# Weaving the first block's products between the last tiles of y, and the second batch's sums into later blocks

## The reference

```
mask   = q_bucket == k_bucket            # 6-bit hash of q and of k
attn   = softmax(where(mask, q @ k.T / 8, -1e9))
x      = attn @ v, put together to 1536 x 512
y      = max(x @ w1, x @ w2, x @ w3) @ moe_w_out      # 1536 x 512
h      = y @ w_in                        # 512 x 2048
g      = h * sigmoid(1.702 * h)
out    = g @ w_out2                      # 1536 x 512
```

## Time and profile before

| | us |
|---|---|
| median of three runs | 686.61 |
| the profiled execution, its own time | 686.38 |
| its span in the trace | 684.6 |
| TensorE busy | 667.9 |
| GpSimd busy | 467.9 |
| VectorE busy | 484.1 |
| ScalarE busy | 345.0 |

### The profile page before, as it was taken

How to read it: one execution, slowest core, us unless ns; L and a number is a source line. 1 busy time by engine, 2 the same in 40 slices (tenths; PEclk the granted TensorE clock), 3 DMA queues, 4 the chain that set the end, 5 groups by cost and what they waited for, 6 DMA issues and landing times.

```text
span 684.6 us, 11930 instructions
## 1 busy us (share of the span) xinstructions
PE 667.9 (98%) x3874; PEld 577.6 (84%) x3874; DVE 484.1 (71%) x971; ACT 345.0 (50%) x755; POOL 467.9 (68%) x539
## 2 busy tenths in 40 slices
PE   7899999999999999999999999899999999999998
PEld 5677776767777789999999999788888898898986
DVE  5877788787878799869788862866655556545454
ACT  3777877777777731011104344554455555544433
POOL 4756756688985899968861438977776667777510
PEclk9999999999999999999999999999999999999999
DMA  4835737548243101111100200322222214222102
GB/s 114 199 85 139 169 91 171 130 116 185 64 117 118 33 31 32 32 32 33 46 25 24 93 1 31 83 71 63 68 86 63 63 46 170 62 73 77 36 1 92
DMA packets 58700, 54.12 MB, mean 79 GB/s; under 512 B 28944, under 2 KB 47632, under 8 KB 58640
## 3 DMA queue, kind: packets, MB, share of 16 engines
q1 hardware_dynamic: 58320, 53.36, 29.0%
q10 hardware_dynamic: 320, 0.01, 0.0%
HBM read 32.51 MB, written 3.15 MB: 52 GB/s over the span
## 4 chain that ended last, share of the span: by engine, by line
PE 83%; POOL 6%; DVE 5%; ACT 2%; issue 2%; DMA 1%; SPq 0%; ACTq 0%; DVEq 0%; POOLq 0%
PE psS L1299 9%; PE psO L1321 9%; PE psR L1307 9%; PE psR L1368 6%; PE psR L1367 6%; PE psR L1369 6%; PE psS L1367 6%; PE psS L1368 6%; PE psS L1369 6%; PE psS L1488 3%; PE psS L1487 3%; PE psS L1486 3%; POOL w_lo L676 2%; PE psR L1268 2%; POOL w_parts L681 2%
## 5 line engine op out<-in xcount | busy, mean ns | idle before, releaser
L547 POOL TENSOR_SCALAR probs<-probs,lone,inv 128x768 f32<-128x768 f32 x96 | 93.7, 982 | 60.7 <-DVE inv L997 60.7
L676 POOL TENSOR_TENSOR w_lo<-w_raw,w_hi 128x256 fp32r<-128x256 f32 x96 | 78.3, 823 | 39.3 <-ACT w_hi L875 38.6
L979 DVE TENSOR_REDUCE neg_max<-psS 128x1 f32<-128x768 f32 x96 | 91.2, 951 | 12.3 <-PE psS L1299 9.1
L732 ACT ACTIVATE probs<-psS,neg_max 128x768 f32<-128x768 f32 x96 | 86.5, 901 | 20.9 <-DVE neg_max L979 20.9
L522 POOL TENSOR_SCALAR w_hi<-w_raw 128x256 fp32r<-128x256 f32 (+1 forms) x79 | 48.6, 618 | 48.4 <-PE psS L1369 26.9
L1307 PE MATMUL psR<-ident,probs 128*128 128x128 f32 x576 | 74.7, 273 | 2.5 <-ACT w_raw L725 0.9
L741 ACT ACTIVATE probs_t<-psR 128x384 f32<-128x384 f32 x128 | 59.5, 491 | 31.3 <-PE psR L1307 31.3
L1307 PEld LDWEIGHTS psR<-ident,probs 128*128 128x128 f32 x576 | 66.6, 140 | 7.1 <-POOL probs L547 3.7
L1321 PE MATMUL psO<-probs_t,v_raw 128*64 128x384 f32 x384 | 68.8, 494 | 0.0
L1202 DVE TENSOR_TENSOR v_raw<-psR,early 128x384 f32<-128x384 f32 x64 | 35.6, 556 | 39.9 <-PE psR L1369 39.2
L1367 PE MATMUL psR<-x_hi,w_hi 128*128 128x384 f32 x160 | 54.2, 339 | 4.6 <-POOL w_lo L676 3.8
(11 more groups left out here) (258 smaller groups left out, 1876.0 us busy)
## 6 DMA issues: line engine op xcount, KB each, us to landing
w_raw<-in_moe_w_in SPq DMA_DIRECT2D x16, 512.0 KB, 3.5
w_raw<-in_moe_w_out SPq DMA_DIRECT2D x32, 256.0 KB, 2.7
w_raw<-in_moe_w SPq DMA_DIRECT2D x9, 512.0 KB, 3.8
h_lo<-w_hi SPq DMA_DIRECT2D x22, 192.0 KB, 3.6
h_hi<-w_hi SPq DMA_DIRECT2D x18, 192.0 KB, 3.4
w_raw<-in_q SPq DMA_DIRECT2D x16, 192.0 KB, 3.4
w_raw<-in_k SPq DMA_DIRECT2D x16, 192.0 KB, 4.1
v_raw<-in_v SPq DMA_DIRECT2D x16, 192.0 KB, 2.5
```

What stands on the lines that cost most here:

```text
L547: pool.tensor_scalar(probs[i % PROBS][:, :], probs[i % PROBS][:, :], lone[:, i % 6:i % 6 + 1], inv[:, i % 6:i % 6 + 1], ALU.add, ALU.mult) ...
L676: pool.tensor_tensor(in2_slot(w_lo, n, which), in2_raw(n, PARTS2[which]), f32(in2_slot(w_hi, n, which)), ALU.subtract).then_inc(in2_split, 1)
L732: act.activation(probs[i % PROBS][:, :].rearrange("p (a b) -> p a b", a=2), psS[i % 2][:, :, 0:HALF], ACT.Exp, bias=neg_max[:, i % 6:i % 6 ...
L979: dve.tensor_reduce(neg_max[:, i % 6:i % 6 + 1], psS[i % 2][:, :, 0:HALF], AX.XY, ALU.min).then_inc(max_ready, 1)
```

## The change

Four things are moved; no computation is added or taken away, the work on each engine is the same.

1. TensorE: of block 0's products, number 0 goes behind tile 12 of y, numbers 1 and 2 behind tile 13, 3 and 4 behind tile 14, 5 and 6 behind tile 15.
2. ScalarE and VectorE: block 0's copies, mixes, sigmoids and gates are placed among the last tiles' `y_hi`, `y_raw_copy` and `y_lo`. The table load for the sigmoid goes from ahead of tile 14 to ahead of tile 10. `in2_hi(1, 4)` now stands behind `g_hi(0, 1)`.
3. ScalarE: `in2_hi(2, 0)` to `in2_hi(2, 3)` stand in block 1, behind `g_hi(0, 3)`, instead of in block 0.
4. Batch 1's `y_sum` go from the ends of blocks 0 and 1 to those of 3 and 4, its `y_sum_lo` from blocks 2 and 3 to 5 and 6, its `y_sum_hi` on ScalarE from blocks 1 and 2 to 4 and 5.

GpSimd's and the DMA queues' programs are the same.

```diff
+    FIRST_MIX = {2 * OUTS * B - 4: (0,), 2 * OUTS * B - 3: (1, 2), 2 * OUTS * B - 2: (3, 4), 2 * OUTS * B - 1: (5, 6)}
 ...
 # ScalarE
+            for n in range(2 * OUTS * B):
 ...
+                if n == 2 * OUTS * B - 6:
+                    act.activation(table_probe[:, :], ident[:, 0:1], ACT.Sigmoid)
+                if n == 2 * OUTS * B - 1:
+                    sigmoid(0, 0)
+                y_hi(n)
+                y_raw_copy(n)
 ...
+                if n == 2 * OUTS * B - 4:
                     first_copy(0)
-                if n + 1 < MIXES:
+            g_hi(0, 0)
+            sigmoid(0, 1)
+            g_hi(0, 1)
+            in2_hi(1, 4)
+            out2_hi(0)
+            out2_hi(1)
+            sigmoid(0, 2)
+            g_hi(0, 2)
+            in2_hi(1, 5)
+            in2_hi(1, 6)
+
+            for n in range(1, MIXES):
+                sigmoid(n - 1, 3)
+                if 1 < n < MIXES - 1:
                     in2_hi(n + 1, 4)
-                if n > 0:
-                    first_copy(n)
-                    g_hi(n - 1, 3)
+                first_copy(n)
+                g_hi(n - 1, 3)
+                if n == 1:
+                    for which in range(5):
+                        in2_hi(2, which)
 ...
-                if n in (1, 2):
-                    for t in T_ORDER2[2 * n - 2:2 * n]:
+                if n in (4, 5):
+                    for t in T_ORDER2[2 * n - 8:2 * n - 6]:
                         y_sum_hi(1, t)
 ...
 # VectorE
-            for n in range(2 * OUTS, 2 * OUTS * B):
+            for n in range(2 * OUTS, 2 * OUTS * B - 1):
                 y_lo(n)
 ...
+                if n == 2 * OUTS * B - 3:
+                    mix(0, 0)
+                    mix(0, 1)
+            mix(0, 2)
+            mix(0, 3)
+            mix(0, 4)
+            gate(0, 0)
+            y_lo(2 * OUTS * B - 1)
+            g_lo(0, 0)
+            gate(0, 1)
+            mix(0, 5)
+            g_lo(0, 1)
+            mix(0, 6)
+            gate(0, 2)
+            g_lo(0, 2)
 ...
-                if n < 2:
-                    y_sum(1, 2 * n)
-                    y_sum(1, 2 * n + 1)
-                elif n < 4:
-                    y_sum_lo(1, 2 * n - 4)
-                    y_sum_lo(1, 2 * n - 3)
+                if n in (3, 4):
+                    y_sum(1, 2 * n - 6)
+                    y_sum(1, 2 * n - 5)
+                elif n in (5, 6):
+                    y_sum_lo(1, 2 * n - 10)
+                    y_sum_lo(1, 2 * n - 9)
 ...
 # TensorE, at the end of the loop over y's tiles
                 mm.then_inc(y_ready, 1)
+                for which in FIRST_MIX[n] if n in FIRST_MIX else ():
+                    up2(0, which)
```

More of the change, by code:

```diff
@@ L883, in out2_hi @@
                 act.activation(w2_parts[:, g % W2_SLOTS, 0, :], out2_raw(g), ACT.Copy).then_inc(out2_hi_made, 1)
[L885 to L896, removed]
             def first_copy(n):
@@ L926, in copy_result @@
                 act.activation(result[tile_], acc[tile_], ACT.Copy).then_inc(result_copied[0], 1)
-            for n in range(MIXES):
-                if n > 0:
-                    sigmoid(n - 1, 3)
+            for n in range(2 * OUTS * B):
                 if n == 0:
-                    first_copy(0)
-                if n + 1 < MIXES:
-                    in2_hi(n + 1, 4)
-                if n > 0:
-                    first_copy(n)
-                    g_hi(n - 1, 3)
+                    act.wait_ge(h_lo_made, 2 * UPS)
+                if n == 2 * OUTS:
+                    act.wait_ge(h_lo_made, 2 * UPS * B)
+                if n == 2 * OUTS * B - 6:
[4 more added lines that the diff above has]
+                y_raw_copy(n)
+                if n in (2 * OUTS, 2 * OUTS + 1):
+                    for t in T_ORDER2[2 * (n - 2 * OUTS):2 * (n - 2 * OUTS) + 2]:
+                        y_sum_hi(0, t)
+                if n == 2 * OUTS * B - 4:
+                    first_copy(0)
+            g_hi(0, 0)
[11 more added lines that the diff above has]
+                if 1 < n < MIXES - 1:
+                    in2_hi(n + 1, 4)
+                first_copy(n)
[3 more added lines that the diff above has]
+                        in2_hi(2, which)
                 if n == FPS2 + 1:
@@ L951, in _ @@
                     sigmoid(n, which)
-                    if 0 < n < MIXES - 2:
+                    if n + 2 < MIXES:
                         in2_hi(n + 2, which + 1)
                     g_hi(n, which)
-                if n == 0:
-                    for which in range(1, 4):
-                        in2_hi(2, which)
                 if n == FPS2:
@@ L1219, in copy_result @@
                 dve.tensor_copy(result[tile_], acc[tile_]).then_inc(result_copied[1], 1)
-            for n in range(MIXES):
-                if n > 0:
-                    gate(n - 1, 3)
+            for n in range(2 * OUTS, 2 * OUTS * B - 1):
+                y_lo(n)
+                if n < 2 * OUTS + 2:
+                    for which in range(2 * (n - 2 * OUTS), 2 * (n - 2 * OUTS) + 2):
+                        y_sum_lo(0, which)
+                if n == 2 * OUTS * B - 3:
[13 more added lines that the diff above has]
+            g_lo(0, 2)
+            for n in range(1, MIXES):
+                gate(n - 1, 3)
                 if n == FPS2 + 1:
                     copy_result(0, COPIES[1][1])
-                if n > 0:
-                    g_lo(n - 1, 3)
+                g_lo(n - 1, 3)
                 if n == FPS2 + 1:
@@ L1425, in _ @@
                     product(n, which)
[L1427 to L1445, removed]
             def up2(n, which):
@@ L1488, in out2 @@
                 pe.matmul(acc[tile_], g_part(n, i, 1)[:, ts(tile_, P)], wh, start=False, stop=last).then_inc(tile_summed, 1)
-            for n in range(MIXES):
+            for n in range(2 * OUTS * B):
+                b, d, j = n // (2 * OUTS), n // 2 % OUTS, n % 2
+                if b == 0 and j == 0:
+                    pe.wait_ge(w_split, ALL_PARTS + d + 1)
+                if n < len(psY):
+                    pe.wait_ge(*product_read(7 * QUADS - len(all_banks) + n))
+                else:
+                    pe.wait_ge(y_lo_made, n - len(psY) + 1)
+                waits = {}
+                if n == 0:
+                    waits = {0: (h_lo_made, 6), 3: (h_lo_made, 7), 4: (h_lo_made, 8), 5: (h_lo_made, 9)}
+                elif n == 1:
+                    waits = {3: (h_lo_made, 10), 4: (h_lo_made, 11), 5: (h_lo_made, 12)}
+                elif n == 2 * OUTS:
+                    waits = {f: (h_lo_made, 2 * UPS + 2 * f + 2) for f in range(UPS)}
+                mm = three_terms(psY[n % len(psY)][:, 0:HALF], [
+                    (w_hi[:, d * S + f * P:d * S + f * P + P], w_lo[:, d * S + f * P:d * S + f * P + P],
+                     h_part(b, f, 0)[:, ts(j, HALF)], h_part(b, f, 1)[:, ts(j, HALF)]) for f in range(UPS)], waits=waits)
+                mm.then_inc(y_ready, 1)
+                for which in FIRST_MIX[n] if n in FIRST_MIX else ():
+                    up2(0, which)
+            for n in range(1, MIXES):
                 for which in range(7):
                     up2(n, which)
-                    if n > 0:
-                        for u in range(sum(OUT_SPREAD[:which]), sum(OUT_SPREAD[:which + 1])):
-                            out2(n - 1, u)
+                    for u in range(sum(OUT_SPREAD[:which]), sum(OUT_SPREAD[:which + 1])):
+                        out2(n - 1, u)
             for u in range(len(OUT_UNITS)):
```

## The result

| | before | changed |
|---|---|---|
| median, us | 686.61 | 689.99 |
| profiled execution, us | 686.38 | 690.5 |
| its span, us | 684.6 | 688.7 |
| first matmul of y to the end of the span, us | 312.8 | 316.4 |

Ratio 1.0046, 95% interval 1.0031 to 1.0061 (5 runs against 5): the changed kernel is slower. The last row of the table leaves out what comes before the change. The first matmul of y stands at 371.79 in the trace before and at 372.28 after, 0.49 us later, and up to 374.01 in a kernel whose instructions up to there are the same; so 0.5 of the 4.1 us between the two spans isn't the change's.

A forecast was written before the change was run, and what follows sets the result against it. TensorE, busy 667.9 of 684.6 us, bounds, with GpSimd's chain setting the time from block 2. +3.6 at block 2, -2.6 in blocks 2 to 4, +2.55 behind: +3.6 us, median 690.2 us, range 688.2 to 692.8.

The forecast's parts named there:

- End of y: Last tile of y, behind five of block 0's products: ends 5.2 us later, at 427.15; GpSimd starts at 427.4.
- Block 1's start: Block 1's first product, waiting for mix(0, 5): at 431.1, 1.1 us earlier than before (0.7 to 1.7).
- The pair: GpSimd's two out2_lo, held by ScalarE's new order: end at 435.2, taking 2.54 us.
- The chain to block 2: GpSimd from the end of both out2_lo to block 3's sum s2: 16.0 us against 19.4 before.
- The decisive term: Block 2's first product: at 454.3 against 450.74, 3.6 us later.
- the stall at w_out2: First out2 unit in block 1 waits for GpSimd: new 3.1 us stall, largely covered by the next, so not added.
- Blocks 2 to 4: No sums at these blocks' ends, so 2.6 us of delay come back; block 5 starts at 501.3.
- The later sums: Batch 1's sums at the ends of blocks 3 to 6: three losses of 0.85 us, 2.55 us in all.
- the rival of 0.28: The clock falls a second time, behind the stall at block 2: 1.7 us more, 691.9 us; chance 0.28.
- The faster rival: GpSimd makes up its delay, block 2 starts at 450.9 and later sums are hidden: 684.2 us; chance 0.07.

The follow-up runs named there:

- experiment 5: Changed kernel with ScalarE's in2_hi(n + 2, 1) to (n + 2, 3) set behind the three g_hi of block n; 686.52 us.
- experiment 4: Kernel before with ScalarE's in2_hi(n + 2, 1) to (n + 2, 3) set behind the three g_hi of block n; 683.91 us.
- 6: Changed kernel with GpSimd's parts 9 to 11 put in late_sum, so they wait for tile 13 of y, not tile 15; 690.51 us.
- 7: Changed kernel with GpSimd's parts 9 to 11 in late_sum and six ScalarE in2_hi and out2_hi parts ahead of the last tile's y_hi; 686.28 us.
- 2: Kernel before with only batch 1's sums moved, to blocks 3 to 6; 685.99 us.
- 9: Kernel before, not woven, with ScalarE's in2_hi behind block n's g_hi and batch 1's sums in blocks 3 to 6; 681.80 us.
- 3: Changed kernel with batch 1's sums back at the ends of blocks 0 to 3; 692.03 us.
- 8: Changed kernel with late_sum slots, ScalarE parts before last y_hi, in2_hi behind g_hi, mix(0, 5) earlier, batch 1's sums one per block; 681.13 us.

## Why the prediction was right

The time came out as 689.99 for 690.2, inside 688.2 to 692.8, and the mechanism is the one that was forecast: GpSimd's chain starts late and sets block 2's start. Step by step, with the 0.49 us of start-up taken from the places after:

- *End of y.* Forecast 427.15, GpSimd's waiting instruction at 427.4; measured 427.91 - 0.49 = 427.4.
- *Block 1's start.* 431.1 forecast, 431.04 measured. VectorE's trace shows the course as worked out: `mix(0, 5)` stands behind `y_lo`, `g_lo` and `gate`.

```profile
428.83 0.56 DVE L1150 TENSOR_TENSOR h_lo<-psS,h_lo 128x384 fp32r<-128x384 f32 x1 [2.79 <-ACT probs_t L861]
429.30 0.61 DVE L1218 TENSOR_TENSOR h_lo<-v_raw,h_lo 128x384 fp32r<-128x384 f32 x1
429.84 1.07 DVE L1213 TENSOR_TENSOR v_raw<-v_raw,bits 128x384 f32<-128x384 f32 x1
430.84 0.54 DVE L1208 TENSOR_TENSOR v_raw<-psR,early 128x384 f32<-128x384 f32 x1
```

- *The pair.* 435.2 forecast, 436.0 measured: it took 3.18 us and not 2.54, and the first w_out2 matmul waits 3.8 us where 3.1 were forecast. The cause is only argued, no run tests it: a `g_lo` (0.95) and a `gate` (1.46) of VectorE run beside it, both longer than alone (0.56 and 0.55).
- *The chain to block 2.* 16.0 forecast, 452.39 - 436.49 = 15.9 measured. From there to the product 2.82 (2.83 to 3.3 forecast). Block 2: 454.3 forecast, 454.7 measured. The decisive term was right. That the stall at w_out2 is covered by it was right too, but experiment 5 shows how much it covers: 2.55 of the 4.0 us would be there without it.
- *Blocks 2 to 4* have no gap, as forecast; block 5 starts 0.55 us later than forecast (502.34 - 0.49 = 501.85 for 501.3).
- *The later sums.* Forecast three gaps, each 0.6 us idle and 0.85 lost, 2.55 in all; measured two, 0.93 and 0.62 us idle, a loss of 1.10 and 0.79, 1.9 in all, at blocks 7 and 8. The chain had gained enough to cover block 6 too. This term was 0.65 us too large and made good for the 0.55 too little up to block 5: that the sum fits better than its terms is luck.
- *The clock.* It fell, but in block 1 and for longer than before (0.72 over 434 to 446), where block 2's wait covers it, and not behind block 2: the rival of 0.28 did not happen. Experiment 5 shows what this fall costs when uncovered. I had not priced it at block 1.
- *A reading.* The prediction has `mix(0, 5)` and `mix(1, 5)` as the instructions that end last before 432.24 and 450.74. GpSimd's `w_lo`, which the profile names, ends later by the trace (432.21 and 450.71). But by GpSimd's order these are parts of blocks 2 and 3, which the two products don't read, so the conclusion stands. In experiment 4 block 2 starts at 449.63 without a wait, while GpSimd makes block 3's parts 1 and 2 only from 450.09 on.

Two things that the prediction took from the code were confirmed by runs: that ScalarE's new order holds GpSimd almost as long as the slots do (6 and 7), and that `g_hi` behind a waiting `in2_hi` is what ties TensorE to GpSimd (4 and 5). The faster rival asked for a chain without its losses; the trace shows 1.5 us of losses in 15.9, but its other condition, a pair not held by ScalarE, failed.

## What to carry to other kernels

A bounding engine's gap can be filled with work from behind only if what that work's place released is followed too: here the five moved products delayed the event (the last tile of y) on which another engine's whole queue hung. Follow that queue to its next meeting with the bounding engine. Before that look for the instruction that waits for a slow helper in front of one that the bounding engine needs: here setting that one behind gave more (-3.2 us from y on) than the weave did at its best (-1.2). And where two waits end together, take both away before you judge either.

## What the runs showed of the hardware that I had not expected

The same two waits ahead of block 1 (0.74 and 1.46 us idle, at 429.03 and 431.78 in kernel 4) were followed by half clock in the trace of the kernel before and not in those of kernels 2, 4 and 9. So whether a short pair of stalls costs the clock 1.6 us more isn't fixed by the program; a difference of 1.6 us between two kernels with such stalls can come from it. The runs of the kernel before agree: their mean granted clock lies between 0.993 and 1.000, though a mean doesn't tell the place.

And the start-up before y varies by up to 2.9 us (371.15 to 374.01) between traces of kernels whose instructions are the same up to there, which is why small differences are read from a place behind it. A part of this goes with the clock: in five traces (the changed kernel, 2, 3, 6 and 8) the granted clock is 0.95 over the first 32 us, and y starts at 372.28 to 374.01; in the other seven it is 1.00, and y starts at 371.15 to 372.16.
